# Splitting and reordering copies, gathers and small set-up work in an attention, expert and dense kernel

## What is computed

```
attention: q, k, v of 4 batches x 8 heads x 576 positions x 64
  q, k = rotate(q), rotate(k)            # by cos and sin of the position
  p = softmax(q @ k.T / 8);  x = p @ v   # x: 2304 tokens x 512
experts: logits = (x/|x|) @ (emb/|emb|).T / tau      # 8 experts
  e = argmax(logits);  y = gate * relu(x @ w1[e]) @ w2[e]   # 512 -> 1024 -> 512
dense: h = y @ w_in;  out = (h - tanh(h)) @ w_out           # 512 -> 2048 -> 512
```

## Time and profile before

| | us |
|---|---|
| median of three runs | 1074.72 (1074.65 to 1074.92) |
| the profiled execution | 1074.65 |
| its span, first to last instruction | 1072.9 |
| TensorE matmuls busy | 986.1 (92%) |
| VectorE busy | 597.2 (56%) |
| ScalarE busy | 582.5 (54%) |
| GpSimd busy | 424.6 (40%) |
| mean granted TensorE clock | 0.979 of full |

### The profile page before, as it was taken

One profiled execution on the slowest core, in us unless ns is written; L12 is line 12 of the kernel. 1 busy time (PEld: TensorE's weight loads), 2 busy tenths in 40 slices (PEclk: granted clock), 3 DMA queues, 4 the chain that ended last, 5 costly groups with the idle time before them and its releaser, 6 DMA issues. The chain is left out here.

```text
span 1072.9 us, 18569 instructions
## 1 busy us (share of the span) xinstructions
PE 986.1 (92%) x5624; PEld 875.1 (82%) x5625; DVE 597.2 (56%) x1196; ACT 582.5 (54%) x1276; POOL 424.6 (40%) x228
## 2 busy tenths in 40 slices
PE   2899999999998399999999949999999999999996
PEld 2799899899997278888888837889989898898985
DVE  5577777777776751111111116776666666666664
ACT  2577777777776542232222226665665666655553
POOL 2998878888710249479967011210000000000000
PEclk9999999999999599999999979999999999999999
DMA  8767666565732455324431022420000000000001
GB/s 242 185 192 196 175 157 167 168 185 168 253 109 70 155 210 177 118 82 147 143 111 60 21 79 83 119 75 30 1 29 0 0 29 0 29 0 0 30 1 30
DMA packets 57202, 107.99 MB, mean 101 GB/s; under 512 B 18240, under 2 KB 23872, under 8 KB 54848
## 3 DMA queue, kind: packets, MB, share of 16 engines
q1 hardware_dynamic: 49552, 89.61, 28.4%
q0 software_dynamic: 3440, 11.27, 3.5%
q10 hardware_dynamic: 4160, 6.44, 1.7%
HBM read 61.89 MB, written 17.03 MB: 74 GB/s over the span
## 5 line engine op out<-in xcount | busy, mean ns | idle before, releaser
L1620 PE MATMUL hd_ps<-y_hi,w_hi 128*128 128x384 f32 x384 | 131.7, 343 | 8.2 <-DVE g_sb L1791 8.2
L1689 ACT ACTIVATE mag<-hd_ps 128x384 f32<-128x384 f32 x96 | 47.4, 493 | 152.7 <-PE hd_ps L1620 150.2
L1620 PE MATMUL hd_ps<-y_hi,w_lo 128*128 128x384 f32 x384 | 129.9, 338 | 0.0
L1620 PE MATMUL hd_ps<-y_lo,w_hi 128*128 128x384 f32 x384 | 129.8, 338 | 0.0
L990 DVE TENSOR_REDUCE neg_max<-ps 128x1 f32<-128x576 f32 x144 | 108.0, 750 | 29.9 <-PE ps L573 27.3
L1006 DVE TENSOR_TENSOR pt_lo<-ps,pt_hi 128x512 fp32r<-128x512 f32 x144 | 99.2, 689 | 44.4 <-ACT pt_hi L765 42.7
L765 ACT ACTIVATE pt_hi<-ps 128x512 fp32r<-128x512 f32 x144 | 86.9, 605 | 60.0 <-PE ps L620 58.7
L1638 PE MATMUL o_ps<-w_hi,g_hi 128*128 128x512 f32 x288 | 114.8, 399 | 2.2 <-DVE g_lo L1800 2.2
L1800 DVE TENSOR_TENSOR g_lo<-g_sb,g_hi 128x384 fp32r<-128x384 f32 x96 | 53.6, 558 | 112.8 <-ACT g_hi L1704 112.8
L1638 PE MATMUL o_ps<-w_lo,g_hi 128*128 128x512 f32 x288 | 114.4, 397 | 0.0
L573 PE MATMUL ps<-k_st,q_st 128*128 128x288 f32 x512 | 95.4, 312 | 20.6 <-DMA q_st<-qk_split 18.6
(11 more groups left out here) (220 smaller groups left out, 2344.8 us busy)
## 6 DMA issues: line engine op xcount, KB each, us to landing
k_st<-qk_split SPq DMA_DIRECT2D x64, 288.0 KB, 4.5
raw_qk<-in_qk SPq DMA_DIRECT2D x14, 1152.0 KB, 5.4
w_stage<-in_w SPq DMA_DIRECT2D x28, 512.0 KB, 3.4
q_st<-qk_split SPq DMA_DIRECT2D x60, 144.0 KB, 3.4
y_rows<-y_row ACTq DMA_DIRECT2D x20, 256.0 KB, 2.1
raw_v<-in_v SPq DMA_DIRECT2D x32, 128.0 KB, 2.2
w_stage<-in_w_in SPq DMA_DIRECT2D x8, 512.0 KB, 3.5
token_rows<-in_w_out SPq DMA_DIRECT2D x16, 256.0 KB, 3.0
```

Of the source, the lines that this page charges most:

```text
L1620: op = nc.tensor.matmul(hd_ps[f % 2][:, 0:G], w[:, c, cols], y[:, c, :], start=c == 0 and h == 0, stop=c == DC - 1 and h == 2)
L1689: nc.scalar.activation(mag[r][:], hd_ps[r][:, 0:G], ACT.Abs).then_inc(mag_done, 1)
```

## The change

The change has these parts.

- The stacks: `hi` and `lo` become two tensors, and so do the two K stacks. A K copy takes one part, so there are eight of 144 KB for each pair; `stack_q` issues the two heads within a part instead of the two parts within a head. `STACKS` grows from 8 to 12 copies.
- The start: the embedding is loaded behind the tables; VectorE squares it between K and Q of pair 0 and clamps its norm after Q; ScalarE's root stands behind the Q copies; VectorE's eight small operations move in among the maxima of pair 0, behind the fifth, and VectorE scales the fold table behind the last instead of GpSimd.
- The first expert's second half of weights is issued by SyncE in the attention block, when the squares of x are done.
- Gathers: twelve (1 to 12) at the start of the experts block, eight (13 to 20) before the first split, and the first split is in the loop of the others. In the dense block the gathers no longer wait for TensorE.

```diff
-AHEAD = 5
+AHEAD = HELD - 8
...
-        STACKS = 8 * 16
+        STACKS = 12 * 16
...
-        k_st = [[put(f"k_st{r}{u}", [P, 2, S], F32R) for u in range(2)] for r in range(2)]
-        k_hh, k_ll = ([[k_st[r][u][:, part, :] for u in range(2)] for r in range(2)] for part in range(2))
+        k_hh = [[put(f"k_hh{r}{u}", [P, S], F32R) for u in range(2)] for r in range(2)]
+        k_ll = [[put(f"k_ll{r}{u}", [P, S], F32R) for u in range(2)] for r in range(2)]
...
             def stack_k(r, landed=None):
                 landed = landed or (stack_in[r], stack_in[r])
                 for u in range(2):
-                    both = qk_split[u * DH:(u + 1) * DH, :, 1, :].bitcast(F32)
+                    rows = slice(u * DH, (u + 1) * DH)
                     for half in range(2):
-                        sp.dma_start(k_st[r][u][half * DH:(half + 1) * DH, :, :].bitcast(F32), both).then_inc(landed[u], 16)
+                        to = slice(half * DH, (half + 1) * DH)
+                        sp.dma_start(k_hh[r][u][to, :].bitcast(F32),
+                                     hi[rows, 1, :].bitcast(F32)).then_inc(landed[u], 16)
+                        sp.dma_start(k_ll[r][u][to, :].bitcast(F32),
+                                     lo[rows, 1, :].bitcast(F32)).then_inc(landed[u], 16)
 
             def stack_q(r):
-                for u in range(2):
-                    for half in range(2):
-                        sp.dma_start(q_st[r][u][half * DH:(half + 1) * DH, u * TAIL:u * TAIL + S].bitcast(F32),
-                                     qk_split[u * DH:(u + 1) * DH, half, 0, :].bitcast(F32)).then_inc(stack_in[r], 16)
+                for half, part in enumerate((hi, lo)):
+                    to = slice(half * DH, (half + 1) * DH)
+                    for u in range(2):
+                        sp.dma_start(q_st[r][u][to, u * TAIL:u * TAIL + S].bitcast(F32),
+                                     part[u * DH:(u + 1) * DH, 0, :].bitcast(F32)).then_inc(stack_in[r], 16)
...
             sp.wait_ge(x_stored, 16 * 2 * (B + 1))
+            sp.wait_ge(sq_done, T)
+            for c in range(UP, CHUNKS):
+                sp.dma_start(early_half(rows, c), weight_chunk(a["w1"], a["w2"], expert, c)).then_inc(second_half[c - UP], 16)
...
-            act.dma_start(emb_sb[:], a["emb_t"].rearrange("(c p) e -> p c e", p=P)).then_inc(emb_in, 16)
             act.dma_start(cos_sb[:, 1, :], a["cos"]).then_inc(tables_in, 16)
             act.dma_start(sin_sb[:, 1, :], a["sin"]).then_inc(tables_in, 16)
+            act.dma_start(emb_sb[:], a["emb_t"].rearrange("(c p) e -> p c e", p=P)).then_inc(emb_in, 16)
...
+            dve.wait_ge(tables_in, 32)
+            rope_first(1, first_k_in, first_k_mult, first_k_done)
+
             dve.wait_ge(emb_in, 16)
             nc.vector.tensor_tensor(emb_sq[:], emb_sb[:], emb_sb[:], ALU.mult).then_inc(emb_squared, 1)
 
-            dve.wait_ge(tables_in, 32)
-            rope_first(1, first_k_in, first_k_mult, first_k_done)
+            dve.wait_ge(table_scaled, 2)
+            rope_first(0, first_q_in, mult_done, rope_done)
             dve.wait_ge(emb_summed, 1)
             nc.vector.tensor_scalar(emb_n[:, 0, :], norm_ps, 1e-30, None, ALU.max).then_inc(emb_clamped, 1)
...
             for i in range(TILES):
                 maximum(0, 0, i)
+                if i == MIX:
+
+                    dve.wait_ge(tau_in, 16)
+                    chain(nc.vector.reciprocal(inv_tau, tau_sb))
+                    dve.wait_ge(emb_root, 1)
+                    newton(chain, nc, emb_n[:, 2, :], emb_n[:, 1, :], emb_n[:, 0, :], emb_n[:, 3, :])
+                    chain(nc.vector.tensor_scalar(emb_n[:, 4, :], emb_n[:, 2, :], inv_tau, None, ALU.mult))
+
+            dve.wait_ge(consts_in, 16 * 6)
+            by_emb = emb_n[:, 4, :].unsqueeze(1).to_broadcast([P, PB, E])
+            nc.vector.tensor_tensor(fold_sb[:, :, 0:E], fold_sb[:, :, 0:E], by_emb, ALU.mult)
+            nc.vector.tensor_tensor(fold_sb[:, :, FW:FP], fold_sb[:, :, FW:FP], by_emb, ALU.mult).then_inc(fold_scaled, 1)
...
             for f in range(KF):
                 if GT + f < T - 2:
-
-                    pool.wait_ge(g_used, f + 1)
                     gather(GT + f)
```

More of the change, by code:

```diff
@@ L146, in attention @@
         pt_lo = put("pt_lo", [P, FULL + 1, MAIN], F32R)
+        lo_at = w_at + 4 * (10 * S + 4 * WIDE + (FULL + 1) * WIDE_PT)
         v_split1 = put("v_split1", [P, TILES + 2, 2 * DH], F32R)
@@ L152, in attention @@
         probs0 = put("probs0", [P, FULL, 2 * S])
-        qk_split = put("qk_split", [P, 2, 2, S], F32R)
-        hi, lo = (qk_split[:, part, :, :] for part in range(2))
+        hi = put("qk_hi", [P, 2, S], F32R)
+        lo = put("qk_lo", [P, 2, S], F32R)
         cos_sb = put("cos_sb", [P, 2, S])
@@ L206, in attention @@
         below = table[:, P + MT + E * T + E:TABLE]
-        tile_eq = spots(nc, w_at + 3 * SET // 4)("tile_eq", [P, T, MT])
+        tile_eq = spots(nc, lo_at)("tile_eq", [P, T, MT])
         have, index, key, first_row = order[:, 0, :], order[:, 1, :], order[:, 2, 0:E], order[:, 3, 0:E]
@@ L830, in _ @@
             for u in range(2):
-                for half in range(2):
-                    act.dma_start(q_st[0][u][half * DH:(half + 1) * DH, u * TAIL:u * TAIL + S].bitcast(F32),
-                                  qk_split[u * DH:(u + 1) * DH, half, 0, :].bitcast(F32)).then_inc((first_a, stack_in[0])[u], 16)
+                for half, part in enumerate((hi, lo)):
+                    to = slice(half * DH, (half + 1) * DH)
+                    act.dma_start(q_st[0][u][to, u * TAIL:u * TAIL + S].bitcast(F32),
+                                  part[u * DH:(u + 1) * DH, 0, :].bitcast(F32)).then_inc((first_a, stack_in[0])[u], 16)
+            act.wait_ge(emb_clamped, 1)
+            nc.scalar.activation(emb_n[:, 1, :], emb_n[:, 0, :], ACT.Sqrt).then_inc(emb_root, 1)
             act.wait_ge(sums_set, 1)
@@ L1172, in _ @@
         def _(sp):
-            expert = sp.value_load(plan[0:1, FIRST, 0:1], min_val=0, max_val=E - 1)
-            for c in range(UP, CHUNKS):
-                sp.dma_start(early_half(rows, c), weight_chunk(w1, w2, expert, c)).then_inc(second_half[c - UP], 16)
             def load_set(before, source):
@@ L1196, in _, with split_set @@
         def _(pool):
-            def split_set(before, slot, between=None):
+            def split_set(before, slot):
                 for c in range(CHUNKS):
-                    if between:
-                        between(c)
                     if c == 0:
@@ L1232, in _ @@
                 gather(t)
-            def two_more(c):
-                for t in range(AHEAD + 2 * c, min(AHEAD + 2 * c + 2, HELD)):
-                    gather(t)
             pool.wait_ge(one_set, 1)
@@ L1241, in _ @@
             last = pool.value_load(plan[0:1, LAST, 0:1], min_val=0, max_val=E - 1)
-            with pool.If(last > 0):
-                slot = pool.value_load(plan[0:1, SLOT, 1:2], min_val=0, max_val=1)
-                split_set(0, slot, two_more)
-            with pool.If(last < 1):
-                for t in range(AHEAD, HELD):
-                    gather(t)
-            for t in range(AHEAD + 2 * CHUNKS, HELD):
+            for t in range(AHEAD, HELD):
                 gather(t)
-            with pool.Fori(1, 3) as before:
+            with pool.Fori(0, 3) as before:
                 next_set(before)
```

15 lines of the change are left out of this document (removed).

## The result

The changed kernel takes 1083.52 us (median, 1081.81 to 1085.83) where the kernel before takes 1074.68: 1.0085 times as long, with a 95% interval of 1.0065 to 1.0104. It is slower, and the forecast of 1075.2 was wrong. Two things stood out at once. The single times lie over 4 us apart, against less than 1 in the few of the kernel before (in the longer series further down, its times spread over 2.2 to 4.4 us as well), and the profiled execution took 1088.51 us (span 1086.7), 13.8 of span more than before.

What follows compares the result with a forecast made beforehand. TensorE was taken to set the pace from 39 us, and one chain from the sine table to pair 1's stack before that. Terms -0.5 + 0.05 + 0.5 + 0.5 = +0.55 on 1074.65 gave 1075.2 us, range 1072.4 to 1078.8.

Steps and rivals of the forecast that it cites:

- The order on VectorE: At the start, moving eight small operations and two fold scalings among pair 0's maxima was claimed hidden with 0.8 us cover.
- Tables before the embedding: At the start, both tables issue 0.49 us earlier; taken as -0.5 us, bounds 0 and -0.8.
- The square between K and Q: At the start, the embedding's square replaces the clamp on VectorE; taken as +0.05 us, bounds -0.2 and +0.2.
- The root behind the Q copies: At the start, ScalarE's root and table load add 1.5 us but are ready at 22.7, needed at 23.5: hidden.
- K stacks: Pair 1's stack on SyncE, eight K copies instead of four: taken as +0.5 us, bounds -0.2 and +3.3.
- Rival 1: Slower: each SyncE stack issue costs 0.92 us whatever is pending, +3.3 at pair 1, giving 1078.0 or 1086; 12%.
- Steady state: In later pairs, a stack of 10 to 10.5 us fits in 13.8 us, covered by 3.3: no cost.
- Second half of the weights: At the expert stage's entry, the earlier 2 MB delay gather 0: taken as +0.5 us, bounds 0 and +1.2.
- rival 3: Slower: at the expert stage's entry, gather 0 queues behind the whole 2 MB, +3.5 us, giving 1078.2; 8%.
- Nothing either way: In the expert stage, twelve gathers at once, eight before the first split and one split loop cost or gain nothing.
- Zero; +1.9 if they suffer: At the dense entry, unpaced gathers cost zero, since the first three are issued first; +1.9 us if they are slowed.

Runs made afterwards that it cites:

- the three altered parts: Changed kernel with the eight small operations early and fold scalings on GpSimd, second-half weights issued in the expert stage, dense gathers paced: 1073.74 us, 0.9994.
- b_one_loop: Kernel before with dense gathers unpaced, one loop for the splits, five x gathers first and the rest in a row behind the first chunks: 1090.79 us, 1.0147.
- b_scale_late: Kernel before with the eight small operations behind the fifth maximum of pair 0 and both fold scalings on VectorE: 1083.95 us, 1.0090.
- a_half_back: Changed kernel with the second half of the first expert's weights issued in the expert stage again: 1089.26 us, 1.0129.
- a_paced: Changed kernel with the dense gathers paced again by TensorE's progress: 1084.63 us, 1.0087.
- after_again: Changed kernel measured once more, unaltered, on another chip: 1092.60 us, 1.0154 against the kernel before.
- b_half: Kernel before with only the second half of the first expert's weights issued in the attention stage: 1076.21 us, 1.0014.

## Why the prediction was wrong

**The order on VectorE** is the step that failed, in the sentence that the eight operations and two scalings "delay the sixth by about 1.1, and through the two score banks the last by about 0.4", hidden with 0.8 us of cover. It priced them at 0.18 each, from the earlier trace rows, where GpSimd stands still. In their new place GpSimd is busy with hardly a gap, show its operations of 2.65 us, and VectorE's operations wait for their end: three that had taken 0.57 together took 6.4. Alone the step cost 9.4 us. It appeared among the rivals in no form.

The Trainium skill, "SBUF — State Buffer", section "SBUF: two separate sides", states this: one pair of ports is shared by VectorE and GpSimd, as an exclusive lock for the whole instruction, and a VectorE operation with two inputs in SBUF, or in a fast mode, takes it. The runs agree, down to the exceptions: the reciprocal (0.20, at 35.25) and the maxima from PSUM (0.76) run beside GpSimd unhindered. The prediction cites that page for another matter and passed over this one.

**Tables before the embedding**, forecast -0.5: the direction was right, the size wrong both ways. K starts 2.56 earlier, far past the bound of -0.8. The square between K and Q, called 0.05, then waits up to 3.73 for a load that the same edit put last. The new order of the start by itself, wait included, is worth -1.9; with that wait removed 2.3 more came on top of the three altered parts (1073.74 to 1071.44). The forecast looked at the square's length and not at what it waits for.

**The root behind the Q copies** was hidden, as forecast: its table load and root end at 21.44 in the changed kernel, and the first exponential starts at 23.25.

**K stacks**, forecast +0.5 (-0.2 to +3.3): the low end holds. In the changed kernel the issues of pair 1 are 0.51 to 0.60 long and 0.64 apart, and 0.60 is the median of the later pairs too. The twelfth starts at 29.58 + 11 x 0.64 = 36.6 and lands 2.9 later: 9.9 us, against 9.96. Rival 1, an issue at 0.92, is out. **Steady state**: a pair is busy as before to 0.03 us, as forecast.

**Second half of the weights**, forecast +0.5 with an upper bound of 1.2: the mechanism was right and the term mis-sized. Alone it measured +1.4; in the stretch it is +1.7 to +2.0 in five profiles. Gather 0's landing (6.0) is 2.6 later than quiet and its reading has no more than 0.7 of slack. It is rival 3's mechanism at about half the price given there (3.5).

**Gathers**: the two steps, "Nothing either way" and "Zero; +1.9 if they suffer", failed together and only together. Dense unpaced alone is indeed nothing (1074.66), twelve ahead with pacing too (1070.35 and 1069.81); both at once cost 5.8. The steps asked when gathers land, and they land in time; what is late is ScalarE's reading of what TensorE has finished.

**What stays open**: why blocks are seen late. Shown is that it takes long rows of gathers issued by GpSimd without a wait, and that one row of sixteen in the dense stage, after x gathers in short rows, does not do it, though it brings the same bytes at the same pace, while a single row of sixteen in the first tiles does (`b_one_loop`). Whether the issuing or the bytes matter isn't shown. Nor is it shown whether TensorE's signal is held up or ScalarE's own program; that the late instruction is each time one that waits for TensorE speaks for the signal. The eight profiles with a late signal at the entry have one thing in common: the last late reading starts 1.4 to 3.0 us after GpSimd's last issue of the row has ended (in the changed kernel 658.40 and 655.81), and no block finished after that is read late. How the first row acts on the second, 250 us later, isn't known.

The clock adds to each delay. In the changed kernel the granted clock is 0.50 (1.2 GHz) from 634.6 on and rises to 1.00 (2.4 GHz) at 648.2 as before; then, after TensorE had stood idle from 652.0 because of the late signals, it is 0.50 again from 655.0, for 10.3 us, where the kernel before has 3.4. The windows of the kernel before at that place, and of the changed kernel:

```profile
641.90:648.70 6.80, 4.53 (x26) 4.21 (x26) 2.73 (x6) 4.69 (x10) 0.00 (x0) 1.00 0.00 1
648.70:652.10 3.40, 3.40 (x11) 3.16 (x10) 2.92 (x7) 1.00 (x3) 0.00 (x0) 0.50 0.29 77
```

```profile
634.60:648.20 13.60, 3.87 (x16) 3.33 (x17) 2.68 (x7) 4.47 (x9) 9.85 (x10) 0.50 0.70 216
648.20:655.00 6.80, 3.81 (x22) 3.49 (x20) 1.23 (x3) 1.88 (x4) 4.97 (x7) 1.00 0.71 211
655.00:665.30 10.30, 7.61 (x20) 6.45 (x21) 4.70 (x11) 5.58 (x12) 0.81 (x1) 0.50 0.30 88
...
726.70:730.10 3.40, 3.40 (x13) 3.40 (x12) 3.20 (x8) 0.07 (x1) 1.32 (x2) 0.50 0.02 5
```

The last row, a second fall in a stretch where TensorE is busy throughout, is half of 3.4 = 1.7 us of work lost, out of the 2.8 us that the profile loses behind the entry. The profiles of `b_scale_late` and `a_half_back` have it too, at 722 and 728; those of `a_paced` and `after_again`, whose bodies start as late, do not. Nothing here says why.

## What to carry to other kernels

Before moving small VectorE operations, look at what GpSimd does beside their new place: their price isn't their own length but the rest of the GpSimd operation that they meet, one after the other, 0.17 us idle and up to 2.54 us beside it here. Of a load that is moved back in a queue, ask who waits for it, and in which order that engine takes its work; and of a wait that only paces transfers, ask what it keeps apart before taking it out, in runs enough to see a spread. An edit that doesn't pay as it stands (separate K tensors, tables first) can pay once the step behind it uses it.

## What the runs showed of the hardware

- A VectorE tensor_tensor or tensor_scalar of 128x8 elements, 0.17 us alone, takes up to 2.54 us beside a 2.6 us GpSimd operation and ends within 0.04 us of it.
- While GpSimd issues 16 gathers in a row, 1.25 us apart, ScalarE can see TensorE's finished block about 8 us late (why is open, and the dense row alone does not do it): with both gather edits its first reading comes 11.1 us after the block's first product (652.71 and 641.6), and 3.1 in the kernel before. By their times it happened in 7 of 9 executions of one kernel, and the times of two others spread over 8.6 and 10.8 us.
- A gather issued while the 2 MB of a second half of weights are queued lands in 6.0 us (6.1 in `b_half`) instead of 3.4 (3.8 in `a_half_back`).
